# Agent attention on one Trainium2 core: agents, scores and exponentials padded to 80 columns and read once, where 49 columns were read twice

## What is computed

```python
def _attn_ref(q, k, v, agents):            # q, k, v: 12480 x 128; agents: 49 x 128
    scale = 1.0 / np.sqrt(q.shape[-1])
    def sm(a, b):
        s = scale * (a @ b.transpose(0, 2, 1))
        s = s - s.max(-1, keepdims=True)
        e = np.exp(s)
        return e / (e.sum(-1, keepdims=True) + 1e-09)
    agent_v = sm(agents, k) @ v            # 49 x 128
    return sm(q, agents) @ agent_v         # 12480 x 128
x = moe(attn)     # h = x @ w_in; g = h if h>=1, 0 if h<=-1, else (h+1)^2/4; g @ w_out
out = moe2(x)     # h = x @ w_in; g = s*relu(h)^2 + b;                       g @ w_out
```

## Time and profile before

| what | value |
|---|---|
| median of 3 runs | 1121.38 us (1121.28 to 1121.69) |
| the profiled execution, its own time | 1120.79 us |
| its span, first to last instruction | 1118.8 us |
| TensorE busy (matmuls) | 1100.6 us, 98% of the span |
| DVE, ACT, POOL busy | 917.9, 917.0, 839.9 us |
| the start, up to the first matmul of the loop | 65.4 us |
| mean granted clock of TensorE | 0.997 of full speed |

### The profile page before, as it was taken

The page is one execution under the profiler, slowest core; times in us unless marked ns, Lnnn a source line. Parts: engine busy times, 40 slices in busy tenths (PEclk is TensorE's granted clock), DMA queues, the critical chain, the costliest instruction groups (busy, mean ns, idle before and its releaser), DMA issues.

```text
span 1118.8 us, 18754 instructions
## 1 busy us (share of the span) xinstructions
PE 1100.6 (98%) x5188; PEld 918.1 (82%) x5188; DVE 917.9 (82%) x1461; ACT 917.0 (82%) x1744; POOL 839.9 (75%) x1225
## 2 busy tenths in 40 slices
PE   9898999999999999999999999999999999999998
PEld 9876888888888888888888888888888888888886
DVE  4768888888788888888788888888788878888876
ACT  2256888888888888888888888888888888888887
POOL 2346887888788887888788787788788788788770
PEclk9899999999999999999999999999999999999999
DMA  9600000000000000000000000000000000000000
GB/s 375 272 1 1 1 19 19 1 19 19 1 18 19 0 18 19 0 18 19 1 18 19 0 19 19 0 18 19 1 18 19 0 19 19 0 18 9 10 1 19
DMA packets 11837, 30.42 MB, mean 27 GB/s; under 512 B 1568, under 2 KB 8192, under 8 KB 11264
## 3 DMA queue, kind: packets, MB, share of 16 engines
q1 hardware_dynamic: 11776, 29.79, 7.4%
HBM read 23.40 MB, written 6.39 MB: 27 GB/s over the span
## 4 chain that ended last, share of the span: by engine, by line
PE 91%; DVE 3%; ACT 3%; issue 2%; DMA 0%; ACTq 0%; SPq 0%; DVEq 0%
PE ps_y L478 8%; PE ps_h L515 8%; PE ps_h L517 8%; PE ps_h L516 8%; PE ps_o L551 8%; PE ps_o L553 8%; PE ps_y L480 8%; PE ps_o L552 8%; PE ps_h L496 8%; PE ps_y L479 8%; PE ps_h L497 7%; PE ps_y L413 2%; PE ps_h L397 2%; PE ps_job L375 1%; ACT sb_g_hi L614 1%
## 5 line engine op out<-in xcount | busy, mean ns | idle before, releaser
L914 POOL TENSOR_TENSOR sb_g_lo<-sb_square,sb_g_hi 128x500 fp32r<-128x500 f32 x380 | 485.0, 1276 | 31.7
L780 DVE SCALAR_TENSOR_TENSOR ps_h<-sb_square,ps_h 128x500 f32<-128x500 f32 (+1 forms) x400 | 272.0, 680 | 110.1 <-ACT sb_square L606 108.0
L614 ACT ACTIVATE sb_g_hi<-ps_h 128x500 fp32r<-128x500 f32 (+1 forms) x400 | 235.9, 590 | 122.8 <-DVE ps_h L780 110.9
L762 DVE SCALAR_TENSOR_TENSOR sb_g_lo<-ps_h,sb_g_hi 128x500 fp32r<-128x500 f32 (+1 forms) x400 | 270.8, 677 | 37.6 <-ACT sb_g_hi L614 28.1
L767 DVE TENSOR_SCALAR sb_below<-ps_h 128x500 f32<-128x500 f32 (+1 forms) x384 | 259.0, 675 | 10.0 <-PE ps_h L497 9.3
L636 ACT ACTIVATE sb_relu<-ps_h 128x500 f32<-128x500 f32 (+1 forms) x400 | 235.3, 588 | 18.7 <-PE ps_h L517 9.6
L645 ACT ACTIVATE sb_square<-sb_relu 128x500 f32<-128x500 f32 (+1 forms) x400 | 246.8, 617 | 0.6
L606 ACT ACTIVATE sb_square<-sb_below 128x500 f32<-128x500 f32 (+1 forms) x384 | 237.6, 619 | 0.4 <-DVE sb_below L767 0.3
L912 POOL TENSOR_SCALAR sb_g_hi<-sb_square 128x500 fp32r<-128x500 f32 x380 | 229.1, 603 | 0.0
L911 POOL TENSOR_TENSOR sb_gate<-sb_ones 1x1 f32<-1x1 f32 x380 | 70.7, 186 | 156.2 <-ACT sb_square L645 154.8
L478 PE MATMUL ps_y<-sb_g_hi,sb_w_out_hi 128*128 128x500 f32 (+1 forms) x400 | 160.8, 402 | 5.4 <-DVE sb_g_lo L762 3.1
(11 more groups left out here) (95 smaller groups left out, 1279.9 us busy)
## 6 DMA issues: line engine op xcount, KB each, us to landing
sb_q_ring<-in_q SPq DMA_DIRECT2D x25, 250.0 KB, 2.7
sb_kv_ring<-in_k SPq DMA_DIRECT2D x12, 512.0 KB, 8.0
sb_kv_ring<-in_v SPq DMA_DIRECT2D x12, 512.0 KB, 15.0
out<-sb_out_ring SPq DMA_DIRECT2D x24, 250.0 KB, 2.1
sb_w_stage<-in_moe_w_out SPq DMA_DIRECT2D x2, 1024.0 KB, 15.7
sb_w_stage<-in_moe_w_in SPq DMA_DIRECT2D x1, 1024.0 KB, 16.0
sb_w_in<-in_moe_w_in SPq DMA_DIRECT2D x1, 1024.0 KB, 16.2
out<-sb_out_ring SPq DMA_DIRECT2D x1, 240.0 KB, 2.0
```

What stands on the lines that cost most here:

```text
L614: nc.scalar.activation(g1_hi[:, place % SPLIT_RING, 0:width(n)], h1_bank(n, place), ACT.Relu).then_inc(g1_hi_ready, 1)
L762: nc.vector.scalar_tensor_tensor(g1_lo[:, slot, 0:columns], h1_bank(n, place), 0.0, as_f32(g1_hi[:, slot, 0:columns]), ALU.max, ALU.subtra ...
L780: nc.vector.scalar_tensor_tensor(h, square1[:, place % WORK_RING, 0:width(n)], 1.0, h, ALU.min, ALU.add).then_inc(g1_summed, 1)
L914: nc.gpsimd.tensor_tensor(g2_lo[:, place % SPLIT_RING, 0:columns], square, as_f32(hi), ALU.subtract).then_inc(g2_split, 1)
```

## The change

Three tensors get 80 columns. The agents come from the host padded with zeros from 49 to 80 columns. The score matmuls read all 80 once. ACT copies all 80 columns of each tile to `a_scores`, whose tiles now lie 80 elements apart, and whose tile count goes from 104 to 98. Maximum, subtraction, exponential and sum still touch only the first 49 of each 80 (`block_scores`). The v matmuls read 80 columns, the last 31 of which are zeros. The matmul of the sums reads 49 columns once.

```diff
-TWICE = 2
+COLS = 80
+N_AGENTS = 49
@@
-        agents_t = sb("agents_t", [C, n_agents])
+        agents_t = sb("agents_t", [C, COLS])
@@
-        a_scores = sb("a_scores", [128, BLOCKS * KV_TILES, n_agents], where=start_only)
+        a_scores = sb("a_scores", [128, KV_BLOCKS * KV_TILES + LAST_TILES, COLS], where=start_only)
@@
-            return a_scores[0:block_rows(n), n * KV_TILES:n * KV_TILES + block_tiles(n)]
+            return a_scores[0:block_rows(n), n * KV_TILES:n * KV_TILES + block_tiles(n), 0:n_agents]
@@
-        def twice(ap, rows):
-            return ap.rearrange("p (t a) -> p t a", t=1).to_broadcast([rows, TWICE, n_agents])
@@ score_q
-                                   agents_t[:], start=True, stop=True)
+                                   agents_t[:, 0:n_agents], start=True, stop=True)
@@ score_k
-                    mm = pe.matmul(score_banks[g % SCORE_BANKS][0:rows, t * TWICE * n_agents:(t + 1) * TWICE * n_agents],
-                                   keys[:, at:at + rows], twice(agents_t[:], C), start=True, stop=True)
+                    mm = pe.matmul(score_banks[g % SCORE_BANKS][0:rows, t * COLS:(t + 1) * COLS],
+                                   keys[:, at:at + rows], agents_t[:], start=True, stop=True)
@@ sum_exp
-                pe.matmul(o_ps[:, 0:TWICE * n_agents], ones[0:rows, :], twice(a_block[0:rows, n % 2], rows), start=(n == 0),
+                pe.matmul(o_ps[:, 0:n_agents], ones[0:rows, :], a_block[0:rows, n % 2], start=(n == 0),
@@ weigh_v
-                    mm = pe.matmul(y_ps[:, 0:TWICE * n_agents], values, twice(a_scores[0:rows, n * KV_TILES + t], rows),
+                    mm = pe.matmul(y_ps[:, 0:COLS], values, a_scores[0:rows, n * KV_TILES + t],
@@ keep_scores
-                               subs(score_banks[g % SCORE_BANKS][0:rows, 0:tiles * TWICE * n_agents], TWICE * n_agents)[:, :, 0:n_agents]).then_inc(a_scores_kept, 1)
+                               subs(score_banks[g % SCORE_BANKS][0:rows, 0:tiles * COLS], COLS)).then_inc(a_scores_kept, 1)
@@ host
-        "agents": turned(agents, agents.shape[0]),
+        "agents": turned(agents, COLS),
```

More of the change, by code:

```diff
@@ L55, in build_program @@
     n_tokens = k.shape[1]
-    n_agents = agents.shape[1]
+    n_agents = N_AGENTS
     D_FF = w_in1.shape[1]
```

## The result

The changed kernel took 1161.72 us (median of 4 runs, 1160.91 to 1161.82) against 1121.33 us (4 runs, 1120.69 to 1121.69): ratio 1.0359, interval 1.0343 to 1.0376. The prediction was 1121.4 us with a range up to 1125.5. What came is its first rival, the clock that stays low in both stages, priced at 1157. The ratios further down leave out runs over 1.5% above the fastest of their kernel, so single times are given where that matters.

A forecast was written before the change was run, and what follows sets the result against it. TensorE was taken as the bound, busy 98% of the span, paced at the start by weight loads. Terms -0.015 + 0.04 + 0 gave +0.03 us, so 1121.4 us was forecast, range 1119.0 to 1125.5 (0.80).

The forecast's parts named there:

- first rival: Scores and v matmuls: fewer columns leave the clock at 1.2 GHz; 1157 us, or 1141 if only v; chance 0.17.
- The pace of PE: Score and v matmuls: weight columns set the 112 ns interval, moving columns hide behind the weight load; change 0.
- third rival: Score and v matmuls: the interval follows moving columns, 15 ns saved on each of 392; about 1118.4 us; chance 0.03.
- ACT's copies: Score stage: 25 copies of 320 elements instead of 196, 0.43 us each, covered by ACT's idle time; 0 on the path.
- DVE's wider step: Maximum and sum reductions: step of 320 bytes instead of 196, taken as 0; up to +2.5 + 1.6 us; chance 0.04.
- the agents' load: Start of the kernel: 40 KB loaded instead of 24.5 KB, moving everything by 0.04 us.
- second rival: DVE's maximum and sum reductions slowed by the wider step between tiles, up to 1125.5 us; chance 0.04.
- The clock: Score and v stages: clock taken as unchanged; staying at 1.2 GHz in one or both had chance 0.17, 1141 to 1157.
- PE has no idle time in either stage: Score and v stages: argument against a low clock, PE being as busy after the change as before.
- The sum matmuls: Between v blocks: 26 instructions go from 98 columns to 49, a pair stays at 0.22 us; 0.
- the clock rises later: Score and v stages: clock rises four us later in each, v loses two us, scores nothing; 1123.4 us; chance 0.06.

The follow-up runs named there:

- g1: Kernel before with 49 columns read once in scores, v matmuls and sums, filling matmuls, and POOL's w_out1 split moved later: 1155.47 us, ratio 1.0303.
- e5: Changed kernel with 98 columns for only the first nine score groups and first five v blocks with their sums: 1121.82 us, ratio 1.0002.
- p1: Kernel before with one edit, POOL splitting w_out1 only after the first probabilities; transposes stay, no filling: 1116.00 us, ratio 0.9958.
- e7: Kernel before with one edit, the matmul of the sums reading 49 columns once instead of twice: ten runs, 1119.0 to 1145.3 us.
- e1: Changed kernel padded with zeros to 98 columns instead of 80: 1128.49, 1145.73, 1134.46 and 1134.32 us, ratio 1.0142.
- e4: Changed kernel with v matmuls reading the 49 exponentials twice again (98 columns), scores still 80 with zeros: 1151.48 us.
- f2: Changed kernel with filling matmuls at the start and around the maximum, and POOL's w_out1 split moved after the first probabilities: 1116.71 us, ratio 0.9958.
- e2: Changed kernel with the 31 padding columns holding the first 31 agents again instead of zeros: 1144.83 us, one execution.
- e8: Changed kernel with filling matmuls replacing transposes at the start and around the maximum, plus 16 before PE's wait for DVE: 1118.90, 1119.72 and 1140.79 us.
- a0: Changed kernel run once more without edit: 1162.32, 1160.70, 1161.64 and 1137.51 us.
- f1: Kernel before (98 columns) with filling matmuls at the start and around the maximum, and POOL's w_out1 split moved later: 1116.29 us, ratio 0.9954.

## Why the prediction was wrong

**The pace of PE: right.** The interval goes by the weight columns. 49, 80 and 98 moving columns gave v blocks of 1.79, 1.81 and 1.79 us when the clock was up (g1, e5, p1), 3.41, 3.47 and 3.41 when it was down; differences of 0.02 to 0.06 are made up by the sums beside them: a block with its pair takes 2.01 us up (1.79 with 0.22, 1.81 with 0.20 in e5) and 3.84 down (3.47 with 0.37, 3.41 with 0.43 in g1). The third rival, 36 cycles gained, is refuted.

**ACT's copies, DVE's wider step, the agents' load: right.** 426 ns against 430 worked out, 814 against 822 and 829; the first k block let the scores begin at 5.06, before at 5.09. The second rival is refuted.

**The clock: wrong, by the chance given.** The mechanism stood as the first rival, with 0.17. Its price was near: 16 us were forecast for the scores and 15.9 measured, 20 for the v stage and 22.4. Missing from it were the slow work behind the last block, 2.3 us, and the 2.6 us in the loop, together the 5 us between 1157 and 1161.7. The step that failed is the one that weighed it: "PE has no idle time in either stage". That is true, before and after, and it does not decide: g1 lost the clock with no wait ahead of the fall, and the changed kernel did not gain it in 98 us, in which PE waited 1.1 us in all and not at all during the scores. The prediction knew that the trace held a rise on 98 columns only, and that 80 were outside it; it should have made the open case and the forecast about equally likely, and the range wide enough for both. The advice of the Trainium skill (TensorE: Matmul & The Clock Gate, Part 1) to avoid idle gaps, quoted there as speaking for no change, agrees with the fall around the maximum, and the traced execution of p1 shows it work; that keeping PE busy is enough for a rise, these runs contradict.

**The sum matmuls: wrong.** "A pair stays at 0.22 us", so 0. Their time did stay. But by e7 alone, halving their columns costs up to 23 us in some executions and nothing in others. An edit costed by its duration had a second effect, through the clock, on everything around it. How the 22.4 us of the v stage divide between the sums and the 80 columns, no run shows.

**The case "the clock rises later": wrong as sized.** I gave it four us a stage. Where it happened in a trace it lasted four blocks (e1), eight (e4) and all twelve (e7).

What is shown: the loss is the clock's, since the changed matmuls take no longer once it is up (e5, f2); 80 columns kept it (e2's scores, e5, e8, f2); in the scores they did not raise it where 98 did (changed kernel, e4, a0); halving the sums alone delays or prevents the rise in the v stage (e7). Zeros and the single reading do not prevent a rise (e1); whether scores of 80 columns without zeros would have raised it was not run, since e2's began with the clock up. What is only inferred: that e1 and e4 were late for the same reason as e7, the sums. What stays open, beside the division of the v stage, is why the first stage begins at full pace in some executions, as in e1, e2 and e7, and not in others, as in the kernel before and the changed one; the same 13 transposes stand ahead of it each time.

## What to carry to other kernels

A matmul whose moving columns hide behind its weight load is not free to be trimmed: the hidden columns may be what brings the clock up, and the bill comes as half speed on all that follows. Ask of such an edit, and of small matmuls beside it, whether the clock must rise or only be kept during it, and count instructions per microsecond, since neither the busy share nor the granted clock of the first stretch shows the loss. Better than either width is to remove the gap in which the clock falls: moving one step of another engine gave 5 us at 98 columns (p1). With that move and filling ahead of the scores, 80 and 98 columns came to the same (f1, f2); the move alone was not run at 80, and its scores would still have to find the clock up.

## What the runs showed of the hardware

- Rise and keeping were different: 80 columns ran at full pace from 5 to 27 us in e2 and from 49 us to the end of the v blocks in e5, and at half pace through 41.9 us of scores in the changed kernel, with PE busy in all of them.
- The clock fell during back-to-back matmuls of 49 columns, from 20 instructions in 2 us to 11 in 1.8 us (g1).
- The rise can differ between executions of one program by as much as the whole stage: 1119.0 to 1145.3 us over ten runs of e7.
- A DVE instruction on SBUF alone stood 3.66 us until POOL's 4.53 us instruction on SBUF had ended; without it, it took 0.21 us. DVE's reductions beside the same instruction took 0.83 us as ever. The Trainium skill (SBUF — State Buffer, Who interferes with whom) says just this: a DVE instruction with two SBUF inputs waits for a GpSimd instruction that reads SBUF, a reduction does not. The rows of both kernels agree; I had read L707's 3.66 us as given, and it was worth more than the change could be.
